# Zero-padded rows of v, another order of the score tiles, and thresholds by tensor_reduce in an attention-and-mixing kernel

## What is computed

```python
def _attn_ref(q, k, v, tau) -> np.ndarray:      # q, k, v: (8, 8, 576, 64) f32
    scale = 1.0 / np.sqrt(q.shape[-1])
    scores = scale * np.matmul(q, k.transpose(0, 1, 3, 2))
    thresh = np.max(scores, axis=-1, keepdims=True) - tau
    scores = np.where(scores >= thresh, scores, -1000000000.0)
    scores = scores - np.max(scores, axis=-1, keepdims=True)
    attn = np.exp(scores)
    attn = attn / (np.sum(attn, axis=-1, keepdims=True) + 1e-09)
    return np.matmul(attn, v).astype(np.float32)
...
    k = np.maximum(xk @ w_k, 0.0)               # first layer, x: (8, 576, 512)
    v = k * k @ w_v
    r = 1.0 / (1.0 + np.exp(-(xr @ w_r)))
    return (r * v).astype(np.float32)
...
    val = x @ w_val                             # second layer, gate: convolution of 5 taps
    return (gate * val @ w_out).astype(np.float32)
```

## Time and profile before

| | us |
|---|---|
| median of 3 runs (1294.01 to 1294.61) | 1294.31 |
| profiled execution, its own time | 1294.74 |
| its span, first to last instruction | 1292.6 |
| mean granted clock of PE over the span, as a share of full speed | 0.996 |

### The profile page before, as it was taken

How to read it: one execution, slowest core, us unless ns; L and a number is a source line. 1 busy time by engine, 2 the same in 40 slices (tenths; PEclk the granted TensorE clock), 3 DMA queues, 4 the chain that set the end, 5 groups by cost and what they waited for, 6 DMA issues and landing times.

```text
span 1292.6 us, 29348 instructions
## 1 busy us (share of the span) xinstructions
PE 1276.2 (99%) x9396; PEld 1132.8 (88%) x9396; DVE 896.2 (69%) x1992; ACT 835.3 (65%) x2015; POOL 335.3 (26%) x371
## 2 busy tenths in 40 slices
PE   7999999999999999999999999999999999999999
PEld 7778777777777777779999999999999999999998
DVE  4788778777787787768576656657655766566554
ACT  4888888888888888875554454445445544544432
POOL 2465555666655555443000000000000000000000
PEclk8999999999999999999999999999999999999999
DMA  6456666665666665512001100110111011001001
GB/s 151 113 149 150 166 158 162 157 149 150 150 158 167 162 167 138 124 42 85 27 10 36 35 17 30 36 36 1 36 44 33 5 36 35 17 28 36 17 1 42
DMA packets 136824, 105.12 MB, mean 81 GB/s; under 512 B 91424, under 2 KB 108064, under 8 KB 136736
## 3 DMA queue, kind: packets, MB, share of 16 engines
q1 hardware_dynamic: 135232, 103.40, 31.1%
q10 hardware_dynamic: 1504, 0.62, 0.2%
HBM read 54.56 MB, written 19.02 MB: 57 GB/s over the span
## 4 chain that ended last, share of the span: by engine, by line
PE 95%; ACT 2%; DMA 1%; DVE 1%; issue 1%; SPq 1%; ACTq 0%; DVEq 0%
PE score_ps L956 31%; PE score_ps L1043 16%; PE aux_ps L489 14%; PE aux_ps L572 13%; PE score_ps L530 12%; PE aux_ps L1027 8%; ACT k_raw L601 1%; PE aux_ps L499 1%; DMA q_all<-q_lo 1%; ACT probs L619 0%; DMA rem_nat<-in_k 0%; DVE probs L690 0%; DVE neg_max L685 0%; DVE kk_lo L1174 0%; SPq L339 0%
## 5 line engine op out<-in xcount | busy, mean ns | idle before, releaser
L685 DVE TENSOR_REDUCE neg_max<-score_ps 128x1 f32<-128x576 f32 x288 | 212.0, 754 | 73.4 <-PE score_ps L530 73.4
L690 DVE SCALAR_TENSOR_TENSOR probs<-score_ps,threshold,probs 128x576 f32<-128x576 f32 x288 | 228.1, 809 | 43.5 <-ACT probs L619 42.9
L530 PE MATMUL score_ps<-k_all,q_all 128*128 128x288 f32 x1280 | 235.2, 314 | 5.1 <-DVE probs L690 4.2
L956 PE MATMUL score_ps<-xm_hi,w_lo 128*128 128x288 f32 x768 | 225.9, 294 | 1.7 <-ACT r_tanh L1140 1.7
L956 PE MATMUL score_ps<-xm_hi,w_hi 128*128 128x288 f32 x768 | 226.6, 295 | 0.0
L956 PE MATMUL score_ps<-xm_lo,w_hi 128*128 128x288 f32 x768 | 226.4, 295 | 0.0
L619 ACT ACTIVATE probs<-score_ps,neg_max 128x576 f32<-128x576 f32 x288 | 212.5, 738 | 0.0
L530 PEld LDWEIGHTS score_ps<-k_all,q_all 128*128 128x128 f32 x1280 | 179.9, 191 | 12.0 <-DVE probs L690 6.4
L601 ACT ACTIVATE probsT<-aux_ps 128x512 f32<-128x512 f32 x288 | 164.1, 595 | 36.6 <-PE aux_ps L489 32.2
L489 PE MATMUL aux_ps<-ident,probs 128*128 128x128 f32 x1280 | 185.6, 276 | 0.7 <-ACT probsT_rem L601 0.6
L489 PEld LDWEIGHTS aux_ps<-ident,probs 128*128 128x128 f32 x1280 | 149.3, 141 | 18.9 <-ACT probsT L601 15.2
(11 more groups left out here) (88 smaller groups left out, 2398.8 us busy)
## 6 DMA issues: line engine op xcount, KB each, us to landing
k_all<-k_all SPq DMA_DIRECT2D x31, 320.0 KB, 4.4
q_all<-q_lo SPq DMA_DIRECT2D x62, 160.0 KB, 3.7
recip_rows<-recip_scratch SPq DMA_DIRECT2D x64, 144.0 KB, 4.4
x_scratch<-x_out SPq DMA_DIRECT2D x32, 288.0 KB, 2.1
out<-y SPq DMA_DIRECT2D x36, 256.0 KB, 2.0
k_all<-k_all SPq DMA_DIRECT2D x31, 288.0 KB, 3.5
v_nat<-in_v SPq DMA_DIRECT2D x32, 256.0 KB, 3.6
qk_nat<-in_q SPq DMA_DIRECT2D x63, 128.0 KB, 2.7
```

Source lines behind the costliest of these rows:

```text
L530: last = nc.tensor.matmul(ps[:, half, 0:HALF], query(h, i, par), kk[par][:, at:at + HALF], start=(n == 0), stop=(n == len(terms) - 1))
L685: nc.vector.tensor_reduce(neg_max[:, i:i + 1], scored(i), mybir.AxisListType.XY, ALU.max, negate=True).then_inc(max_ready, 1)
L690: nc.vector.scalar_tensor_tensor(tile_halves(i), scored(i), threshold[:, i:i + 1], tile_halves(i), ALU.is_ge, ALU.mult, accum_out=row_sum[ ...
L956: last = nc.tensor.matmul(ps, w, m, start=(n == 0), stop=(n == 3 * len(terms) - 1))
```

## The change

- **v.** The remainders of the two heads lay in one block of `v_nat`, head 0 on partitions 0 to 63 and head 1 on 64 to 127, and pv read 64 rows for each. Now they lie in `v_rem`, one block for each head, whose other 64 rows GpSimd sets to zero once at the start. pv reads all 128 rows of `probsT_rem`, in which both heads' rows lie. The identity matrix and the first load of v are ordered behind that memset.
- **Order.** Scores go 3 1 2 4 0 8 6 7 5 (before: 1 0 2 4 3 5 7 6 8), and all plans are new. A tile's slot is now its turn in that order modulo 3, and the waits on masks follow it.
- **Thresholds.** `neg_max` has two columns for each tile: the negated maximum and |tau|, written once. DVE forms thresholds of two tiles at a time (`thr0` to `thr3`; `thr4` for the ninth) as the negated sum of the two columns. ACT's instruction for each tile is gone, and exp waits only for max; mask waits for exp and for the thresholds.
- **Sums.** `row_sum` has a second column with 1e-9, and `sum` is a reduction of the two into `divisor`.

```diff
 PE_PLAN = steps("""
-    probs5- scores1 k0 kq0 scores0 pv0- q0 scores2 probs6- scores4 rem1- probs4- scores3 probs7-
-    probs8- scores5 probs2 pv1- probs1 scores7 probs0 rem0 scores6 scores8 probs3
+    scores3 kq0 probs2- scores1 k0 pv0- probs4- scores2 q0 scores4 rem1- probs5- scores0 probs1
+    scores8 probs7- probs6- scores6 probs8- probs3 scores7 pv1- probs0 scores5 rem0
 """)
...
+BY_TURN = sorted(SCORE_TURN, key=SCORE_TURN.get)
...
+THRESHOLDS = [range(n, min(n + 2, TILES)) for n in range(0, TILES, 2)]
...
-        v_nat = sb("v_nat", [P, 2, TILES, D])
+        v_nat = sb("v_nat", [P, 2, MIX, D])
+
+        v_rem = sb("v_rem", [P, 2, 2, D])
...
-        neg_max = sb("neg_max", [P, TILES])
+
+        neg_max = sb("neg_max", [P, TILES, 2])
...
-            return score_ps[i % SLOTS][:, :, 0:HALF]
+            return score_ps[SCORE_TURN[i] % SLOTS][:, :, 0:HALF]
...
+            for h in range(2):
+                eng.dma_start(v_rem[REM * h:REM * (h + 1), par, h, :],
+                              heads["v"][it * 4 + (2 * c + h), MAIN:S, :]).then_inc(v_loaded[par], 16)
...
+            nc.gpsimd.memset(v_rem[:], 0.0).then_inc(ident_made, 1)
+            pool.wait_ge(ident_made, 3)
...
-                                rows = slice(0, P) if t < FULL else slice(REM * h, REM * (h + 1))
-                                m = probsT[:, t, h, cols] if t < FULL else probsT_rem[rows, cols]
+                                m = probsT[:, t, h, cols] if t < FULL else probsT_rem[:, cols]
+                                values = v_nat[:, cc % 2, h * FULL + t, :] if t < FULL else v_rem[:, cc % 2, h, :]
...
-                        nc.scalar.activation(threshold[:, i:i + 1], neg_max[:, i:i + 1], ACT.Identity,
-                                             bias=tau_down[:, 0:1], scale=-1.0).then_inc(threshold_ready, 1)
+                        turn = MAX_TURN[i]
                         nc.scalar.activation(tile_halves(i), scored(i), ACT.Exp,
-                                             bias=neg_max[:, i:i + 1], scale=1.0).then_inc(exp_done, 1)
+                                             bias=neg_max[:, turn, 0:1], scale=1.0).then_inc(exp_done, 1)
...
+                    elif kind == "thr":
+                        turns_of = THRESHOLDS[i]
+                        group = slice(turns_of.start, turns_of.stop)
+                        dve.wait_ge(max_ready, count(it, cc, TILES, turns_of.stop))
+                        nc.vector.tensor_reduce(threshold[:, group], neg_max[:, group, :], mybir.AxisListType.X, ALU.add,
+                                                negate=True).then_inc(threshold_ready, 1)
...
-                        nc.vector.tensor_scalar_add(row_sum[:, cc % 2, :], row_sum[:, cc % 2, :],
-                                                    1e-9).then_inc(sum_ready, 1)
+                        nc.vector.tensor_reduce(divisor[:], row_sum[:, cc % 2, :, :], mybir.AxisListType.X,
+                                                ALU.add).then_inc(sum_ready, 1)
```

More of the change, by code:

```diff
@@ L35 @@
 PE_PLAN = steps("""
-    probs5- scores1 k0 kq0 scores0 pv0- q0 scores2 probs6- scores4 rem1- probs4- scores3 probs7-
-    probs8- scores5 probs2 pv1- probs1 scores7 probs0 rem0 scores6 scores8 probs3
+    scores3 kq0 probs2- scores1 k0 pv0- probs4- scores2 q0 scores4 rem1- probs5- scores0 probs1
+    scores8 probs7- probs6- scores6 probs8- probs3 scores7 pv1- probs0 scores5 rem0
 """)
 ACT_PLAN = steps("""
-    probs3- probs5- k0 exp8- kq0 exp1 exp0 pv0- q0 probs6- exp2 rem1- probs4- probs7- probs8- exp4
-    exp5 exp3 probs2 pv1- probs1 probs0 exp7 rem0 exp6
+    rem0- kq0 probs2- exp5- exp1 k0 exp3 pv0- probs4- q0 exp2 rem1- probs5- exp4 probs1 exp0 probs7-
+    probs6- probs8- exp6 probs3 exp8 exp7 pv1- probs0
 """)
 DVE_PLAN = steps("""
-    max8- max1 max0 mask8- sum0- recip0- mask1 max2 mask0 max4 mask2 max3 max5 mask5 mask4 mask3 max7
-    max6 mask7 mask6
+    mask7- max5- thr4- max3 max1 mask5- sum0- thr0 recip0- mask1 mask3 max2 max4 thr1 mask2 max0
+    mask4 max8 thr2 mask0 max6 max7 mask8 thr3 mask6
 """)
 PE_DRAIN = steps("""
-    probs5- pv0- probs6- probs4- hidden0 probs7- probs8- hidden1 rem1- hidden2 pv1- hidden3
+    probs2- pv0- probs4- hidden0 probs5- probs7- probs6- probs8- hidden1 rem1- hidden2 pv1- hidden3
 """)
 ACT_DRAIN = steps("""
-    probs3- probs5- exp8- previous4 previous5 pv0- probs6- previous6 previous7 probs4- probs7- probs8- rem1- pv1-
-""")
-DVE_DRAIN = steps("max8- mask8- sum0- recip0- mix4 mix5 mix6 mix7")
-ACT_EXTRA = {"exp2": "previous0 previous1", "probs4-": "previous2", "probs2": "previous3"}
-DVE_EXTRA = {"max4": "mix0", "max5": "mix1 mix2", "max6": "mix3"}
+    rem0- probs2- exp5- previous4 previous5 pv0- probs4- previous6 previous7 probs5- probs7- probs6-
+    probs8- rem1- pv1-
+""")
+DVE_DRAIN = steps("""
+    mask7- max5- thr4- mask5- sum0- recip0- mix4 mix5 mix6 mix7
+""")
+ACT_EXTRA = {"exp2": "previous0 previous1", "rem1-": "previous2", "probs1": "previous3"}
+DVE_EXTRA = {"max4": "mix0", "max8": "mix1 mix2", "max6": "mix3"}
 FIRST_PREPARE = steps("k0 kq0 q0")
@@ L238, in prepared @@
             return 1 + max(number(run, x) for x in FIRST_PREPARE)
-        def load(eng, nat, name, it, c, loaded):
-            eng.dma_start(nat[:, 0:2 * FULL, :].rearrange("p (h t) d -> p h (t d)", h=2),
-                         heads[name][bass.ds(it * 4 + 2 * c, 2), 0:MAIN, :].rearrange(
-                             "h (p t) d -> p h (t d)", t=FULL)).then_inc(loaded, 16)
-            for h in range(2):
-                eng.dma_start(nat[REM * h:REM * (h + 1), MIX, :],
-                             heads[name][it * 4 + (2 * c + h), MAIN:S, :]).then_inc(loaded, 16)
         def load_head(eng, n, name, it, c, h, loaded):
@@ L273, in load_v @@
         def load_v(eng, it, c):
-            load(eng, v_nat[:, c % 2, :, :], "v", it, c, v_loaded[c % 2])
+            par = c % 2
+            eng.dma_start(v_nat[:, par, :, :].rearrange("p (h t) d -> p h (t d)", h=2),
+                          heads["v"][bass.ds(it * 4 + 2 * c, 2), 0:MAIN, :].rearrange(
+                              "h (p t) d -> p h (t d)", t=FULL)).then_inc(v_loaded[par], 16)
+            for h in range(2):
+                eng.dma_start(v_rem[REM * h:REM * (h + 1), par, h, :],
+                              heads["v"][it * 4 + (2 * c + h), MAIN:S, :]).then_inc(v_loaded[par], 16)
         def stack_q(eng, it, c):
@@ L372, in sync @@
             stack_k_first()
+            sp.wait_ge(ident_made, 3)
             load_v(sp, 0, 0)
@@ L677, in vector @@
             dve.wait_ge(tau_steps, 1)
-            nc.vector.tensor_tensor(tau_down[:], tau_neg[:], tau_sb[:], ALU.min).then_inc(tau_steps, 1)
+            nc.vector.tensor_tensor(neg_max[:, :, 1], tau_neg[:].broadcast_to([P, TILES]),
+                                    tau_sb[:].broadcast_to([P, TILES]), ALU.max).then_inc(tau_steps, 1)
+            nc.vector.memset(row_sum[:, :, :, 1], 1e-9).then_inc(tau_steps, 1)
             def run(plan, it, c):
```

35 lines of the change are left out of this document (18 added, 17 removed).

## The result

The changed kernel takes 1297.59 us (median of 18 runs, 1295.72 to 1299.33), the kernel before, run beside it, 1294.67 (18 runs, 1293.72 to 1295.14): a ratio of 1.0023, 95% interval 1.0016 to 1.0030. The forecast was 1294.4 within 1287.5 to 1299. The time lies in the range, but 2.9 us is just beyond the 0.2% that I had called no difference. The sign is slower. The profiled execution took 1297.20, its span is 1295.4 (before: 1292.6), and the mean granted clock of PE is 0.997 of full speed.

The account below looks back on a forecast made before the run. The prediction took a pair's loop of PE work up to recip_T, then SyncE's queue and DMA, as the bound. Periods +0.6, head -0.5, tail 0 gave +0.1 us on 1294.74, less 0.43 to the median: 1294.4, range 1287.5 to 1299.

Parts of the forecast that it names:

- B: Second half of a pair's loop, recip_T to next first scores, in SyncE's queue and DMA engines: stays 9.89 us.
- A: First half of a pair's loop, first scores to recip_T, spent on PE: 7.42 us against 7.40 before.
- Rival 1: Attention stage: the matmul engine's own work is the bound, so 21 us less, 1273 us; chance 8%.
- Padding: Remainder matmuls of v: 0.15 us less for each pv; pv0's saving counts, pv1's is hidden behind recip_T.
- Order in A: First scores to pv0: the new tile order takes 2.22 us instead of 1.98, +0.24.
- Rival 2: First scores to recip_T is shorter than added up, by 0.1 to 0.25 us a pair: 1287 to 1291; chance 17%.
- rival 3: Exp2, waiting for VectorE's max2, holds up recip_T: 0.3 us a pair, +9 us, 1303; chance 10%.
- Rival 4: Idle place at the first scores, 0.7 instead of 0.2 us, lowers PE's clock: over 10 us; chance 3%.
- VectorE's reductions: Five new small reductions a pair on VectorE, 0.65 to 1.4 us, some 1.5 with waits: taken as hidden.
- Head: Stretch before 31.70 us, where VectorE and score slots alternate: -0.5 us, between -1.5 and +1.5.
- The 30 periods: Pair 1's to pair 31's first scores: 0.02 us longer each, +0.6 us in all.
- Tail: Last pair and drain: four pv save 0.6 us, waits grow under VectorE's extra work: 0, between -1 and +1.

Follow-up runs that it names:

- b3: Kernel before with zero-padded rows of v for pv0 alone (pv1 keeps 64 x 64 matmuls): 1290.13 us, ratio 0.9972.
- b4: Kernel before with zero-padded rows of v for pv1 alone (pv0 keeps 64 x 64 matmuls): 1292.98 us, ratio 0.9994.
- b2: Changed kernel with two neighbours in SyncE's queue exchanged, stacking q ahead of fetching the reciprocals back: 1280.64 us, ratio 0.9898.
- a1: Kernel before with the zero-padded rows of v alone, order and thresholds as before: 1288.76 us, ratio 0.9950.
- a4: Changed kernel with the padding undone, 64 x 64 matmuls on the remainder again: 1304.05 us, ratio 1.0071.
- a2_thr: Kernel before with thresholds and sums formed by VectorE, order of tiles and v as before: 1296.33 us, ratio 1.0010.
- d1: Changed kernel with tile 2's transposes moved from behind a pair's first scores to ahead of the next pair's first scores: 1288.20 us, ratio 0.9957.
- c1: Changed kernel with q's stacking ahead of the reciprocals' fetch in SyncE's queue, and the drain's transposes reordered: 1280.27 us, ratio 0.9889.

## Why the prediction was right and where it was wrong

**What bounds the kernel: right.** B is 9.88 on the mean, as in the kernel before (9.91), and b3 and b4 show that work on PE counts in A only. Rival 1 fell: PE's busy time went down by 9.3 us, and nothing of that reached the time. One reading of B was wrong, though: I had called its part in the queue bandwidth and not order. The order of two entries alone brings q's landing from 9.47 to 7.97 us behind SyncE's send, with the same transfers (b2).

**Padding: right.** 0.15 us in each pv, in both directions (a1: A -0.148; a4: +0.163; tail of a4 +0.59). The Trainium skill, TensorEngine Tiling (Array Packing), Key Properties, states that a change of tiling mode drains the engine. The gap at 303.98 and its absence at 307.47 agree; that the change is what costs, and not the 64 x 64 form itself, is argued from the gap's place, and no run separates the two. The advice of the Trainium skill, TensorEngine Tiling (Array Packing), When to Use Tiling, row tiles for 64 rows, does not hold here: with heads side by side in both forms, 128 rows with zeros are 5.9 us faster than 64.

**Order in A: right.** 2.23 against my 2.22 up to pv0, and the order alone moved A by 0.262 against 0.24. **ScalarE: right.** Recip_T stands 0.63 behind exp2 and exp2 directly behind q0's copy. (My 6.56 for the earliest exp2 should read 6.51, 4.94 + 0.81 + 0.76; q0's copy ends later than both.) A is 7.42, as added up; before it is 7.377 on the mean and not the 7.40 of the one pair that I read, so that A grew by 0.04 and not 0.02, and B fell by as much. Rival 2 (A shorter) fell by this, and so did rival 3: max2 ended at 316.47 and q0's copy held exp2 until 316.73, so some 0.26 us were left on VectorE. Rival 4 fell: the granted clock reads 1.00 of full speed from 49.2 us to the end (0.93 ahead of it, 0.997 over the span), in spite of idle times of 0.57 and 0.67 at the first scores (forecast 0.5 to 0.8).

**VectorE's reductions: priced near the lower bound, cover right in the new order only.** They take 0.15 to 0.17 us each, where I had bounds of 0.13 and 0.28, and are hidden in A. In the old order they cost 0.15 of B (a2_thr), by a mask at the first scores that the prediction had put in B's shadow without working it out. The new order without the reductions was not run: that they are hidden there is read from the ends of max2 and of q0's copy.

**Head: inside my bounds, but the gain isn't there** (+0.15 against -0.5, between -1.5 and +1.5). PE waits for masks in the head, here for 2.25 us just before pair 1:

```profile
30.92 0.80 PE L540 MATMUL score_ps<-k_all,q_all 128*128 128x288 f32 x4 [2.25 <-DVE probs L707]
```

**The 30 periods: +0.65 against +0.6, in part by luck.** Pair 1's own period took 17.96 us instead of 17.49, which is 0.47 of the 0.65. It is all in B (10.52 instead of 9.98), where the fetch of the reciprocals held the queue for 2.71 instead of 2.16 us:

```profile
42.46 2.71 SPq L345 DMA_DIRECT2D recip_rows<-recip_scratch  x2
```

The 29 periods behind it differ by 0.006 us each, where I had reckoned 0.02 for all 30 alike. Whether every execution has the long first one isn't known: it is read from one.

**Tail: the mis-sized term.** Forecast 0 (-0.6 for four pv, and waits that grow by as much), measured +2.06, three quarters of the slower span. The -0.6 is real (a4). What I left out is work, not a wait. In the old list probs5 stood ahead of the pair's first scores, and four tiles of the pair before (6, 4, 7, 8) behind them; in the new list six stand behind them (2, 4, 5, 7, 6, 8). In the loop that is free or costs A. In the head the same two groups are missing ahead of pair 1's first scores, and that brings nothing, since PE waits for masks there. In the last pair nothing hides PE's work, and two more groups of four are 2 x 0.35 = 0.70. The rest are waits. PE's timeline in the last pair and the drain:

```profile
552.36 0.78 PE L540 MATMUL score_ps<-k_all,q_all 128*128 128x288 f32 x4
553.34 1.95 PE L582 MATMUL aux_ps<-probsT,v_nat 128*64 128x256 f32 x16 [0.20 <-ACT probsT L610]
...
559.77 0.66 PE L498 MATMUL aux_ps<-ident,probs 128*128 128x128 f32 x4 [0.59 <-ACT probsT_rem L610]
...
562.32 0.77 PE L540 MATMUL score_ps<-k_all,q_all 128*128 128x288 f32 x4
563.30 1.14 PE L498 MATMUL aux_ps<-ident,probs 128*128 128x128 f32 x8 [0.21 <-ACT probsT L610]
564.68 0.80 PE L540 MATMUL score_ps<-k_all,q_all 128*128 128x288 f32 x4 [0.24 <-DVE probs L707]
...
569.27 0.98 PE L498 MATMUL aux_ps<-ident,probs 128*128 128x128 f32 x6
570.99 1.95 PE L582 MATMUL aux_ps<-probsT,v_nat 128*64 128x256 f32 x16 [0.73 <-ACT probsT L610]
...
575.39 1.03 PE L498 MATMUL aux_ps<-ident,probs 128*128 128x128 f32 x8
576.67 1.15 PE L498 MATMUL aux_ps<-ident,probs 128*128 128x128 f32 x8 [0.25 <-ACT probsT L610]
577.57 0.38 PE L974 MATMUL score_ps<-xm_hi,w_lo 128*128 128x288 f32 x1
```

The drain of the kernel before:

```profile
567.07 1.03 PE L489 MATMUL aux_ps<-ident,probs 128*128 128x128 f32 x8
568.54 1.95 PE L572 MATMUL aux_ps<-probsT,v_nat 128*64 128x256 f32 x16 [0.44 <-ACT probsT L601]
...
571.00 1.34 PE L489 MATMUL aux_ps<-ident,probs 128*128 128x128 f32 x8
572.10 0.38 PE L956 MATMUL score_ps<-xm_hi,w_lo 128*128 128x288 f32 x1
```

The one wait that I had named in the earlier trace rows, 0.62 at 558.77, is there still (0.59 at 559.77) and has not grown. New are the two at 563.30 and 564.68: a group of scores lasts 0.61 and eight transposes 0.79 where nothing waits (561.53 to 562.32), but the steps are 0.98 and 1.38, so they cost 0.37 and 0.59. In the drain pv0 waits for probs2's copy: six transposes, 0.58 where nothing waits, take 1.72 up to it, a wait of 1.14, and before eight of them (0.79) took 1.47, a wait of 0.68. That is +0.46. The transposes of four tiles in a row, with two banks, take 1.28 and 0.90, 0.60 over their 2 x 0.79; before, in two groups apart, 1.10 and 0.79 (573.77 to 574.56), 0.31 over: +0.29. Together 0.70 + 0.37 + 0.59 + 0.46 + 0.29 = 2.41; less 0.6 for the padding that is 1.8 of the 2.06, and some 0.25 I haven't assigned. d1 shows that this reading is no mere list: with one group taken ahead of the first scores the wait at pv0 in the last pair goes too, and the tail falls by 0.73, of which 0.35 is the group. c1 took 0.45 from the drain's waits. The other waits weren't tried. The eight kernels with the old order have a tail of 29.8 to 30.7 us, the six with the new one 32.0 to 33.3: it is the order's, not the reductions' (a2_thr even has 0.55 less than before).

So the error was one of method. I worked the loop out group by group and gave the drain, which the new order changes as much, one sentence and a symmetric range of 1 us.
